# Two triangular products of a chunked attention, regrouped so that stacked rows of b and k are one weight load

## The reference

```
state = 0                                   # 40 x 40
for t in range(768):
    y[t]  = r[t] @ state
    Sa    = state @ a[t]
    state = state * w[t] - outer(Sa, b[t]) + outer(v[t], k[t])
```

## Time and profile before

| | |
|---|---|
| median of 3 runs | 1658.83 us (1657.92 to 1666.54) |
| the profiled execution's own time | 1660.92 us |
| its span | 1659.2 us |
| mean granted clock of TensorE | 0.897 |
| PE busy | 1485.5 us (90%) |
| PEld busy | 1154.0 us (70%) |
| DVE busy | 575.1 us (35%) |
| ACT busy | 587.6 us (35%) |
| POOL busy | 292.7 us (18%) |

### The profile page before, as it was taken

How to read it: one execution, slowest core, us unless ns; L and a number is a source line. 1 busy time by engine, 2 the same in 40 slices (tenths; PEclk the granted TensorE clock), 3 DMA queues, 4 the chain that set the end, 5 groups by cost and what they waited for, 6 DMA issues and landing times.

```text
span 1659.2 us, 42935 instructions
## 1 busy us (share of the span) xinstructions
PE 1485.5 (90%) x18793; PEld 1154.0 (70%) x18793; DVE 575.1 (35%) x1107; ACT 587.6 (35%) x1167; POOL 292.7 (18%) x263
## 2 busy tenths in 40 slices
PE   1798888998989883799999999999978999999999
PEld 0687777887878672688888888888734555555556
DVE  5473654646544326000000000000046554554441
ACT  1452543526445322111121121211137455455451
POOL 4423232222422000111111111111141100100000
PEclk9886977869788665799999999999979999999999
DMA  4404132241421117755555555555520100000000
GB/s 108 110 8 111 34 92 59 66 103 46 97 48 41 32 31 234 242 167 182 172 165 189 167 177 177 164 189 166 184 79 24 31 29 24 28 24 8 12 8 20
DMA packets 100695, 159.86 MB, mean 96 GB/s; under 512 B 54624, under 2 KB 68960, under 8 KB 99872
## 3 DMA queue, kind: packets, MB, share of 16 engines
q1 hardware_dynamic: 92928, 131.23, 26.6%
q0 software_dynamic: 7584, 25.90, 5.2%
HBM read 140.21 MB, written 16.88 MB: 95 GB/s over the span
## 4 chain that ended last, share of the span: by engine, by line
PE 58%; issue 1%; DMA 1%; DVE 0%; ACT 0%; POOL 0%; POOLq 0%; DVEq 0%
PE pY L985 14%; PE pY L1127 13%; PE pH L966 12%; PE pH L1114 10%; PE pH L971 4%; PE pH L1117 3%; PE pX L955 1%; PE pX L1102 1%; DMA xs<-x,slot_token 0%; PE pX L956 0%; POOL rows L1093 0%; DMA rows<-results,pos 0%; DVE down L1202 0%; DMA results<-ys 0%; DVE down L1203 0%
## 5 line engine op out<-in xcount | busy, mean ns | idle before, releaser
L985 PE MATMUL pY<-down,hT 128*128 x880 | 245.9, 433 | 0.0
L966 PEld LDWEIGHTS pH<-exT,up 128*128 128x128 f32 x1760 | 207.8, 194 | 11.5 <-issue 1.7
L966 PE MATMUL pH<-exT,up 128*128 128x128 f32 x1760 | 208.3, 277 | 2.5 <-ACT exT L1004 2.5
L1127 PE MATMUL pY<-wout,down 128*128 128x320 f32 x768 | 210.4, 433 | 0.0
L1011 ACT ACTIVATE hT<-pH 128x512 f32<-128x512 f32 x110 | 59.7, 594 | 419.3 <-PE pH L971 419.3
L985 PEld LDWEIGHTS pY<-down,hT 128*128 128x128 f32 x880 | 163.0, 190 | 61.2
L1019 DVE COPY ys<-pY 128x320 f32<-128x320 f32 x55 | 27.0, 491 | 507.3 <-PE pY L985 507.3
L1127 PEld LDWEIGHTS pY<-wout,down 128*128 128x128 f32 x768 | 144.3, 190 | 60.7 <-issue 3.0
L1114 PE MATMUL pH<-mxT,win 128*128 128x512 f32 x384 | 174.8, 609 | 4.9 <-ACT mxT L1156 4.1
L1114 PEld LDWEIGHTS pH<-mxT,win 128*128 128x128 f32 x384 | 74.6, 196 | 93.1 <-issue 84.7
L946 POOL DMA_DIRECT2D results<-ys x55 | 31.8, 577 | 428.5 <-DVE ys L1019 428.5
(11 more groups left out here) (189 smaller groups left out, 2159.3 us busy)
## 6 DMA issues: line engine op xcount, KB each, us to landing
up<-in_moe_w SPq DMA_DIRECT2D x55, 1024.0 KB, 5.3
up_rest<-in_moe_w SPq DMA_DIRECT2D x110, 128.0 KB, 5.2
down<-in_moe_w SPq DMA_DIRECT2D x8, 1280.0 KB, 14.5
results<-ys POOLq DMA_DIRECT2D x55, 160.0 KB
wfr<-in_wdec SPq DMA_DIRECT2D x32, 240.0 KB
kbT<-in_kb SPq DMA_DIRECT2D x16, 480.0 KB
aT<-in_at SPq DMA_DIRECT2D x16, 240.0 KB
uv<-in_vt SPq DMA_DIRECT2D x16, 240.0 KB, 6.5
```

The source lines that it names most:

```text
L966: pe.matmul(pH[t % 2][b][:, c, :], up[t % NU][:, k, f * P:(f + 1) * P], xT[t % 2][:, k, :], start=(c == 0 and k == 0), stop=False, skip_gr ...
L985: m = pe.matmul(pY[t % 2][:, 0:D], hT[t % 2][:, j, :], down[:, bass.ds(e, 1), j, :].rearrange("q n d -> q (n d)"), start=(j == 0), stop=(j ...
L1127: m = pe.matmul(pY[t % 2][:, 0:D], h[g % 2][:, f, j * P:(j + 1) * P], wout[:, f, :], start=(f == 0), stop=(f == FT - 1))
```

## The change

T and M are replaced by TMa and TMb. A token TMa takes the cells with i = 0 and computes both their T and their M products; TMb does so for i = 1. The 64 columns of b and the 64 columns of k are loaded together as 128 weight columns, and a's 64 columns are moved past them once. The upper and lower 64 rows of the result are T and M. Each token now has 12 matmuls instead of 24 (6 chunks, h = 0 and 1). Since both products of a pair lie in one slot, DVE takes a slot with two instructions of 64 partitions and 768 values each, one to `tpow` and one to `mT`.

In the order, TMa_0 TMb_0 stand where T0 stood and TMa_1 TMb_1 where T1 stood; the places of M0 and M1 are gone. In LEAD the four new tokens stand together behind K0. Whatever waited for T or M of a half now waits for TMb of that half.

```diff
-ORDER = """u ST1 N0 s UT1 T0 r N1 u H1 I1 t2_0 s J1 Y1 r T1 u n2_0 s t2_1 r w2_0 u K1 s n2_1 r t4_0 u p0 t4_1 K0 n4_1 s
-n4_0 M0 B0 r w4_0 u w2_1 ST0 s M1 r UT0 w4_1 u n8_0 s ...
+ORDER = """u ST1 N0 s UT1 TMa_0 TMb_0 r N1 u H1 I1 t2_0 s J1 Y1 r TMa_1 TMb_1 u n2_0 s t2_1 r w2_0 u K1 s n2_1 r t4_0 u
+p0 t4_1 K0 n4_1 s n4_0 B0 r w4_0 u w2_1 ST0 s r UT0 w4_1 u n8_0 s ...
-LEAD = """p0 N0 K1 N1 K0 T0 M1 T1 n2_0 M0 n2_1 B0 t2_0 t2_1 ...
+LEAD = """p0 N0 K1 N1 K0 TMa_0 TMb_0 TMa_1 TMb_1 n2_0 n2_1 B0 t2_0 t2_1 ...
...
-                    taken(pool, f"T{half}", g)
+                    taken(pool, f"TMb_{half}", g)
...
-                        for i, h, e, x, z in cells():
-                            a = aT[b3][e:e + D, i, cols(k_, C)]
-                            b = kbT[e:e + D, i, k_, i, :]
-                            k = kbT[e:e + D, i, k_, 1 - i, :]
-                            left, right, q = {"N": (a, b, x), "T": (b, a, x), "M": (k, a, z)}[kind]
-                            m = pe.matmul(out[q:q + 64, h, cols(c, C)], left, right, start=True, stop=True)
+                        if kind == "N":
+                            for i, h, e, x, z in cells():
+                                m = pe.matmul(out[x:x + 64, h, cols(c, C)], aT[b3][e:e + D, i, cols(k_, C)], kbT[e:e + D, i, k_, i, :],
+                                              start=True, stop=True)
+                        else:
+
+                            i = 0 if kind == "TMa" else 1
+                            for h in range(2):
+                                e = slice(64 * h, 64 * h + D)
+                                m = pe.matmul(out[:, h, cols(c, C)], kbT[e, i, k_].rearrange("q s f -> q (s f)"), aT[b3][e, i, cols(k_, C)],
+                                              start=True, stop=True)
...
-                    taken(pe, f"M{half}", g)
+                    taken(pe, f"TMb_{half}", g)
...
-                        taken(pe, f"T{half}", g)
+                        taken(pe, f"TMb_{half}", g)
...
+                elif kind in ("TMa", "TMb"):
+                    i = 0 if kind == "TMa" else 1
+                    x, z = slice(64 * i, 64 * i + 64), slice(64 - 64 * i, 128 - 64 * i)
+                    nc.vector.tensor_tensor(tpow[0][x, :, at_], t[x], over_pairs(mask_un)[x], ALU.mult)
+                    m = nc.vector.tensor_tensor(mT[z, :, at_], t[z], over_pairs(mask_u)[z], ALU.mult)
```

More of the change, by code:

```diff
@@ L33, in wait @@
     eng.wait_ge(s, value)
-ORDER = """u ST1 N0 s UT1 T0 r N1 u H1 I1 t2_0 s J1 Y1 r T1 u n2_0 s t2_1 r w2_0 u K1 s n2_1 r t4_0 u p0 t4_1 K0 n4_1 s
[L41 to L45, removed]
+ORDER = """u ST1 N0 s UT1 TMa_0 TMb_0 r N1 u H1 I1 t2_0 s J1 Y1 r TMa_1 TMb_1 u n2_0 s t2_1 r w2_0 u K1 s n2_1 r t4_0 u
+p0 t4_1 K0 n4_1 s n4_0 B0 r w4_0 u w2_1 ST0 s r UT0 w4_1 u n8_0 s t8_1 r n8_1 u t8_0 V1 p1 s n16_1 n16_0
+w8_0 X1 r H0 u w16_0 s w8_1 I0 r E0 B1 u w16_1 L0 s V0 r E1 u J0 s Y0 L1 r F0 X0 F1 u""".split()
+LEAD = """p0 N0 K1 N1 K0 TMa_0 TMb_0 TMa_1 TMb_1 n2_0 n2_1 B0 t2_0 t2_1 w2_1 n4_0 w2_0 p1 n4_1 B1 t4_1 t4_0 V1 n8_0
+w4_0 t8_1 t8_0 w8_0 n8_1 n16_0 w4_1 n16_1 w16_0 w8_1 V0 L0 w16_1 E0 E1 L1 F0 F1""".split()
 DRAIN = """u s ST1 r u s r u UT1 s r H1 u s r u s r u s r u s I1 r J1 Y1 u UT0 s r H0 u X1 s r u ST0 s I0 r J0 Y0 u s
@@ L339, in wide @@
                 b2, b3 = g % 2, g % 3
-                if kind in ("N", "T", "M"):
+                if kind in ("N", "TMa", "TMb"):
                     pe.wait_ge(a_scaled, 2 * g + 2)
@@ L593, in take @@
                     m = nc.vector.tensor_tensor(dst, t, over_pairs(mask_u), ALU.mult)
[L594 to L597, removed]
+                elif kind == "N":
+                    m = nc.vector.tensor_tensor(n32[:, :, at_], t, over_pairs(mask_ln), ALU.mult)
+                elif kind in ("TMa", "TMb"):
[3 more added lines that the diff above has]
+                    m = nc.vector.tensor_tensor(mT[z, :, at_], t[z], over_pairs(mask_u)[z], ALU.mult)
                 elif kind in ("w2", "w4", "w8"):
```

## The result

The changed kernel took 1697.07 us (median of 4 runs, 1695.77 to 1702.2) against 1658.38 for the kernel before beside it: ratio 1.0254 (1.0208 to 1.0300). Six more runs, taken together with two of the experiments, gave 1.0305 (1.0257 to 1.0354). The two ratios put it 42 to 50 us slower (by medians 39 and 52); 51 were forecast, 1710 us with a range from 1694 to 1724. The profiled execution of after took 1695.77 us, its span 1694.0. From the routing to the end the two traces agree within 3 us; the loss lies in the attention.

The account below looks back on a forecast made before the run. PE's ordered stream was taken to bound the kernel. 7 x (4.6 + 3.4 - 1.3) + 6.5 for LEAD - 2 for issue waits gave +51 us, so 1710 us; range 1694 to 1724 for this case, 1685 to 1740 with rivals.

Parts of the forecast that it names:

- What bounds it: Rounds of ORDER, 83 to 560 us: PE's ordered stream rules, busy 425.3 of 477 us.
- Price of a take: DVE, TMa and TMb slots: two instructions of 0.96 us each, so a slot occupies DVE 1.76 us instead of 0.88.
- Price of a block: PE, new blocks of 24 instructions: stream moves on by 2.56 us at the low clock, 1.43 at the high.
- First site: TMa_0 TMb_0 r N1 u, at the low clock: u starts 4.6 us later a round.
- Second site: TMa_1 TMb_1 u n2_0 s t2_1 r: waits at t2_1 and r cost +3.4 us a round.
- M removed: Old places of M0 and M1 further on in the round: their absence gives -1.3 us a round.
- Instruction supply: PE's issue waits, 32.0 us over 11777 instructions: 672 fewer matmuls and their loads give -2 us.
- The sum: Whole kernel: sites, M removed, LEAD and instruction supply together +51 us, 1710 us; forecast's chance 0.64.
- cheap loads: Rival, new PE blocks: the 128-column load hides or does not slow with the clock; 1686 or 1690 us; chance 0.13.
- The clock's falling once more: Rival, rounds: new idle at t2_1 and thinner stream bring 10 us more low clock a round; 1739 us; chance 0.12.

Follow-up runs that it names:

- two of the experiments: Changed kernel with one take per slot, and with 64-column loads and two takes, run again on one chip with the change: ratios 1.0226 and 1.0147 to the kernel before.
- the first traces: Profiles from the first measuring of the changed kernel beside the kernel before: 1697.07 against 1658.38 us, ratio 1.0254.
- the repeat: The changed kernel, unaltered, measured again on one chip with two experiments, against the kernel before: 1704.00 us, ratio 1.0305.
- the first two experiments: Changed kernel with one DVE take per slot: 1691.73 us; changed kernel with 64-column loads, two takes kept: 1691.85 us.
- the order alone: Kernel before in the new order: old T for TMa, old M for TMb, one take each: 1662.97 us, ratio 1.0043.

## Why the prediction was right, step by step

- **What bounds it.** Right: PE's ordered stream, 83 to 600 us.
- **Price of a take.** Right: 64x768 takes 0.95 to 0.96 us, as 128x768 did.
- **Price of a block.** Right: two blocks take 5.32 us at 1.2 GHz; 2.56 plus 2.77 were forecast. At the high clock two take 2.90 where twice 1.43 and a last instruction make 3.1. That the load is the limit was taken from L461 and L971 and is shown by half the columns moved. L971 could not show it by itself, since it moves 128 columns behind each load and not 64. The 213 ns of one row group and the full overlap of two are both shown by the loads themselves (7 and 14 in 1.61 us).
- **First site.** +4.6 us forecast, 4.6 measured in quiet rounds (7.4 to 12.0). On average over rounds 2 to 7 of the first traces it is 8.6 to 12.1, +3.6, since the kernel before had issue waits in this stretch in some rounds and the changed one, with slower blocks, mostly not.
- **Second site.** +3.4 forecast; t2_1 came 3.0 us later in the last round, the take of w2_0 3.5 in quiet rounds and 3.7 on average over rounds 2 to 7, one of which met the low clock there (9.5 us).
- **M removed.** Mis-sized: -1.3 forecast, -0.8 measured between the two places. A wait for `st` took the place of M1. Yet the whole stretch outside the sites, from w2_0's take to the next N0's, fell from 50.3 to 48.0 us on average over rounds 2 to 6, by 2.3. The other 1.5 us a round were not forecast; no run here separates them.
- **Instruction supply.** Mis-sized: the sum of the issue waits scaled by the number of instructions gave -2 us. They fell from 32.0 to 27.2 us, and to 26.2 in the repeat; with the 64-column loads, as many instructions as before, they were 36.8 and 34.2. So they do not follow the number of instructions alone. That they follow the rate at which PE runs through them is a guess that not all runs bear out (last section).
- **The sum.** +51 forecast; +42 in the first measurement, +50 in the second. Executions of one kernel differ by up to 1.5% with their mean clock: beside the first two experiments the kernel before took 1644.5 us at 0.909 and 1668.1 at 0.892. This spread goes with the clock and not with the issue waits. The time at the low level is twice the span times what the mean clock lacks to 1.00: 299 us for the faster one (span 1642.8), 360 for the slower (1666.4), 61 more. A stretch of the low level loses 0.4 of its length, the prediction's own price (0.93 for 1.56 us), so 61 us lose 24, and the two executions lie 23.6 apart. Likewise the two profiled executions of the changed kernel: 12.7 us apart, 27 us more at the low level (11 us by the same price), issue waits within 1 us of each other. Worked out in the same way, the changed kernel's profiled execution of the first measurement was at the low level for 24 us more than that of the kernel before (366 and 342), no more than its longer first site explains (7 x 3.6). In the second measurement it was 68 us more (383 and 315 on average). The longer first site is 25 to 32 us of that; what remains costs 14 to 17 us, an estimate. The sum had put this term at nothing, so that +50 lies so close to +51 is partly luck.

Rivals: cheap loads would have shown 1.5 us blocks at the low clock; no trace has them. Loads of 128 columns repeat every 213 ns at the low clock with 40 rows (all chunks of one row group) and with 128 rows (L461). The Trainium skill's rule in TensorE: Matmul & The Clock Gate, section LDWEIGHTS, says that rows do not count, and the trace agrees. As a time without a clock the rule does not hold: two blocks took 5.32 us at one level and 2.90 at the other.

The clock's falling once more happened in part: from 83 to 560 us the mean is 0.77 instead of 0.80, and 0.74 in the second trace of the change. In the first trace most of that is the first site, which is at the low clock anyway and became 3.6 us longer a round; in the second it is more, as worked out above. In rounds 2 to 7 of the two traces of the change a rise came before the first site once (round 3 of the second, blocks of 2.84 us), and even there the site took 9.6 us.

## What to carry to other kernels

Joining two small matmuls into one with twice the weight columns saves instructions, not load time. Where loads are the limit, as here, four quadrants of 64 columns beat two row groups of 128 (0.93 and 1.56 us against about 1.6 and 2.8 a block): a load of 128 columns takes twice as long, and two lie side by side instead of four. Count also what takes the result out: the slot shared by two products needed two instructions, and each of 64 partitions cost as much as one of 128 (0.95 us). Where PE's order is fixed, find the token that waits behind these takes; its delay, not the busy time, is the cost.

## What the runs showed of the hardware

Float32 loads of 128 columns repeat every 213 ns at 1.2 GHz within one row group. When two row groups alternate, two loads start together every 213 ns, so they overlap wholly. Loads of 64 columns in four quadrants start four in about 107 ns. The 8.12 us of a block in one row group, 165 ns an instruction, are a mean of the two rhythms and the price of neither.

Waits of PE with no engine behind them ("issue", 83 to 600 us) were 25.9 to 28.3 us in five traces with the 128-column blocks in both halves and the given token order and columns, 34.2 and 36.8 us with the 64-column loads and two takes. But with the tokens spread or half the columns moved they were 23.0 and 20.6 us, and with only half 0 or half 1 in the new form 22.0 and 30.2; in the kernel before and with the order alone 32.0 and 31.3. The 128-column blocks go with fewer such waits; why is open.
